# Fourier part folded along channels, woven into the second batch's output products; identity loaded first; row statistics on ScalarE

## The chip, the core and the metric

The kernel runs on one core of a Trainium2 chip. A core has a matrix engine (TensorE, PE in the rows), VectorE (DVE), ScalarE (ACT), GpSimd (POOL) and SyncE (SP), which here issues all transfers. Each engine takes its instructions in order; they wait for each other through semaphores. TensorE writes to PSUM, eight banks of 512 f32 columns; GpSimd cannot read PSUM. The metric is the device time of one execution in microseconds, lower is better.

## What is computed

Three stages follow each other, for two batches of 768 positions and 512 channels. The first is an attention with hashed buckets (8 heads of 64). The second gates a convolution. The third, which the change touches, is this:

```
gate = sigmoid(causal depthwise convolution of x, 5 taps)
x    = (gate * (x @ w_val)) @ w_out            # "y" in the kernel
X    = real(fft along channels (fft along the sequence (x)))
u    = x + X
un   = (u - mean(u)) / sqrt(var(u) + 1e-6)     # over the 512 channels
out  = u + relu(un @ w_ch1) @ w_ch2            # 512 -> 2048 -> 512
```

The real part of the two transforms is a sum of cosine and sine products: first along the sequence, then along the channels, with tables of cosines and sines as matrices.

## The kernel before

**Products.** Each f32 matrix product is made of three matmuls in the rounded type fp32r: both operands are cut into a high part (a copy that rounds) and a low part (the rest), and high x high, low x high and high x low are summed in PSUM (`three`, L1206, issued by `product`, L1087, so that nearly all matmuls have line L1090). So each operand costs a copy, mostly on ScalarE (`hi_...`), and a subtraction, on VectorE or GpSimd (`lo_...`).

**Stages.** The attention runs in 96 units, with `g` counting from -23 (`FIRST`); in it TensorE makes scores in a ring of three pairs of PSUM banks (L1193 to L1204), which VectorE's `maximum` (L827) frees. VectorE's queue before the first maximum holds a wait for the identity and its conversion to bf16 (L901 to L903). SyncE issues that load at `g == -12` (L471), after the first two sets of operands have been stacked and right after the loads of `qk` 2 and 3. After the attention come `values` (L1209), eight column groups for each batch, and `outputs` (L1223), six row tiles of 12 matmuls for each batch. VectorE multiplies with the gate (`gate_values`, L936) and cuts the low part (`lo_gv`, L927). `outputs` needs the first four `g_lo` of its batch for tiles 0 to 2, and all eight for tiles 3 to 5 (L1226).

**Transforms.** `fold_tile` makes sums and differences of the two sequence halves, for batch 0 on VectorE (L950), for batch 1 on GpSimd (L569); `hi_fold` (L722) and `lo_fold` (L578) cut them. `along_sequence` (L1237) runs eight tiles of 9 matmuls with 386 or 384 columns for a batch, `hi_seq` (L731) and `lo_seq` (L959) cut the spectrum, and `along_channels` (L1253) runs six row tiles of 24 matmuls with 258 or 256 columns. For its first tile it issues three quarters of the work before it waits for the last part of the spectrum (L1260). `add_mixed` (L965) adds the result to y in four pieces and takes `bn_stats`; `variances` (L982) and `inverse_deviations` (L992) give the scale, `normed` (L1007) gives `un`, which TensorE transposes (`turn_un`, L1268) and `hi_un` (L746) and `lo_un` (L1015) cut.

**Order and weights.** The order on each queue is written out: TensorE L1282 to L1304, VectorE L1022 to L1054, ScalarE L754 to L783, GpSimd L611 to L626. The Fourier tables come in 16 chunks that GpSimd cuts (`split_tables`, L599), from the end of the attention on. Then come the 16 chunks of w1: GpSimd cuts chunks 0 to 9 alone (`split_w1`, L602), and of the last six ScalarE makes the high part (`hi_w1`, L775) and GpSimd the low one (`lo_w1`, L605). SyncE loads a chunk when the one two before has been cut (L493), into two buffers. The feed-forward (`feed_block`, L1330) runs four blocks of 16 steps: `hidden`, 12 matmuls of 384 columns, and `project`, 9 of 512. Its first block needs all three `unt_lo`.

## Time and profile before

| | |
|---|---|
| time, median of 3 runs | 714.03 us (714.02 to 714.39) |
| time of the profiled execution | 714.04 us |
| its span, first to last instruction | 712.2 us |
| TensorE busy | 684.7 us, 96% |
| VectorE / ScalarE / GpSimd busy | 388.9 / 243.8 / 203.0 us |
| mean granted TensorE clock | 0.987 of full |

The span is read from the first to the last instruction, so 1.8 us of the execution lie around it. A matmul's recorded duration is longer than its place in the stream, as matmuls overlap: the distance between two starts, the pitch, is what a matmul costs. "Idle before" names what ended an engine's idle time. Several instructions of a kind in a row are merged, with their count behind an x.

### The profile page before, as it was taken

The numbers are of one execution on the slowest core, as the hardware profiler recorded it, in microseconds if no ns is written. First come the engines' busy times: TensorE is split into PE (matmuls) and PEld (weight loads), VectorE is DVE, ScalarE is ACT, GpSimd is POOL, SyncE is SP. The second block draws the span as 40 slices with busy tenths as digits, with TensorE's granted clock in tenths as the row PEclk, the third lists the DMA queues.
The fourth block names the chain that finished last, engine by engine and source line by source line (L and its number), as shares of the span: only waits on it lengthen the run. The fifth ranks groups of instructions, "written<-read, shape, count | busy, mean of one in ns | idle before, by whom it ended". The sixth has DMA issues, their size and how long they took to land.

```text
span 712.2 us, 10036 instructions
## 1 busy us (share of the span) xinstructions
PE 684.7 (96%) x3600; PEld 614.7 (86%) x3600; DVE 388.9 (55%) x621; ACT 243.8 (34%) x376; POOL 203.0 (29%) x193
## 2 busy tenths in 40 slices
PE   3699999999999999999999999999999999999998
PEld 2588888888888888798989999999999999999997
DVE  3566768888888888958745796321222122212112
ACT  2065545555555455654345241111112111211110
POOL 0001323232323233538848965880000000000000
PEclk9699999999999999999999999999999999999999
DMA  5945565555655441212202132330100010001001
GB/s 152 249 134 142 131 173 139 166 149 156 154 157 154 119 123 53 75 39 57 55 30 60 31 90 89 89 90 0 45 0 0 0 44 0 0 0 44 1 1 44
DMA packets 43846, 57.64 MB, mean 81 GB/s; under 512 B 21520, under 2 KB 25872, under 8 KB 43808
## 3 DMA queue, kind: packets, MB, share of 16 engines
q1 hardware_dynamic: 43808, 57.14, 29.0%
q8 instruction: 23, 0.38, 0.2%
q14 instruction: 15, 0.12, 0.1%
HBM read 31.81 MB, written 3.24 MB: 49 GB/s over the span
## 4 chain that ended last, share of the span: by engine, by line
PE 92%; DVE 3%; ACT 1%; DMA 1%; SPq 1%; issue 1%; DVEq 0%
PE psum L1090 74%; PE psum L1175 5%; PE psum L1176 4%; PE psum L1182 1%; PE psum L1183 1%; PE psum L1184 1%; PE psum L1187 1%; PE psum L1188 1%; PE psum L1185 1%; PE psum L1157 1%; DVE max_col L830 1%; PE psum L1278 1%; DMA ident<-in_ident_in 1%; DMA qk_raw<-in_qk 1%; ACT probs L669 1%
## 5 line engine op out<-in xcount | busy, mean ns | idle before, releaser
L1061 DVE SCALAR_TENSOR_TENSOR h_lo<-psum,h_hi 128x384 fp32r<-128x384 f32 x64 | 35.7, 558 | 184.2 <-ACT h_hi L791 184.2
L830 DVE TENSOR_REDUCE max_col<-psum 128x1 f32<-128x768 f32 x96 | 91.2, 953 | 40.8 <-PE psum L1090 40.6
L791 ACT ACTIVATE h_hi<-psum 128x384 fp32r<-128x384 f32 x64 | 31.5, 492 | 215.4 <-PE psum L1090 215.4
L669 ACT ACTIVATE probs<-psum 128x768 f32<-128x768 f32 x96 | 77.6, 809 | 39.8 <-PE psum L1090 39.8
L1090 PE MATMUL psum<-unt_hi,w_hi 128*128 (+1 forms) x256 | 86.9, 339 | 0.0
L1090 PE MATMUL psum<-unt_lo,w_hi 128*128 (+1 forms) x256 | 86.3, 337 | 0.0
L1090 PE MATMUL psum<-unt_hi,w_lo 128*128 (+1 forms) x256 | 85.9, 336 | 0.0
L1090 PE MATMUL psum<-a1k,a1q 128*128 128x384 f32 x192 | 67.9, 354 | 11.8 <-DVE max_col L830 6.7
L1090 PE MATMUL psum<-a1q,a1k 128*128 128x384 f32 x192 | 76.0, 396 | 0.8 <-ACT a2q L657 0.8
L1090 PE MATMUL psum<-w_lo,h_hi 128*128 128x512 f32 x192 | 75.9, 395 | 0.0
L1090 PE MATMUL psum<-w_hi,h_lo 128*128 128x512 f32 x192 | 75.8, 395 | 0.0
L1090 PE MATMUL psum<-w_hi,h_hi 128*128 128x512 f32 x192 | 74.6, 389 | 0.0
L1090 PE MATMUL psum<-a2k,a2q 96*128 96x384 f32 x192 | 67.2, 350 | 0.0
L546 POOL TENSOR_TENSOR vl<-v,vh 128x384 fp32r<-128x384 f32 x16 | 20.5, 1284 | 156.7 <-issue 81.6
L1090 PE MATMUL psum<-a2q,a2k 99*128 99x384 f32 x192 | 65.0, 339 | 0.0
L666 ACT ACTIVATE p_hi<-psum 128x768 fp32r<-128x768 f32 x48 | 39.0, 813 | 65.2 <-PE psum L1090 63.5
L836 DVE TENSOR_TENSOR p_lo<-probs,p_hi 128x768 fp32r<-128x768 f32 x48 | 54.0, 1125 | 3.2 <-ACT probs L669 3.2
L557 POOL TENSOR_TENSOR xT<-sums,rec_b 64x768 f32<-64x768 f32 x16 | 30.0, 1872 | 79.0 <-DMA rec_b<-rec_dram 74.4
L1090 PEld LDWEIGHTS psum<-unt_hi,w_hi 128*128 128x128 f32 x256 | 48.1, 188 | 2.2
L1090 PEld LDWEIGHTS psum<-unt_hi,w_lo 128*128 128x128 f32 x256 | 48.1, 188 | 2.2
L1090 PEld LDWEIGHTS psum<-a1k,a1q 128*128 128x128 f32 x192 | 38.2, 199 | 13.3 <-DVE max_col L830 7.3
L1090 PEld LDWEIGHTS psum<-unt_lo,w_hi 128*128 128x128 f32 x256 | 48.0, 188 | 0.0
(129 smaller groups left out, 1449.6 us busy)
## 6 DMA issues: line engine op xcount, KB each, us to landing
stg_w<-in_w SPq DMA_DIRECT2D x32, 256.0 KB, 2.6
qk_raw<-in_qk SPq DMA_DIRECT2D x16, 384.0 KB, 5.1
a1k<-qk_hi SPq DMA_DIRECT2D x32, 192.0 KB, 3.3
flag_b<-flag_dram SPq DMA_DIRECT2D x16, 384.0 KB, 4.2
a1q<-qk_hi SPq DMA_DIRECT2D x16, 192.0 KB, 2.8
a2q<-qk_hi SPq DMA_DIRECT2D x16, 192.0 KB, 3.5
a1q<-qk_lo SPq DMA_DIRECT2D x16, 192.0 KB, 3.7
a2k<-qk_lo SPq DMA_DIRECT2D x16, 192.0 KB, 3.7
```

The lines of the kernel that those rows point to most:

```text
L546: pool.tensor_tensor(vl[par][:, :].rearrange("p (t d) -> p t d", d=P), split_tiles(v1[par][:, :]), bits(vh[par][:, :]).rearrange("p (t d) ...
L557: pool.tensor_tensor(xT[rows, slot * S:(slot + 1) * S], sums[par][rows, :], rec_b[rows, :], ALU.mult).then_inc(x_ready, 1)
L666: act.activation(halves(p_hi[k % PHBUF][:, 0:S]), ring("st", i), ACT.Exp, scale=SCALE).then_inc(p_hi_ready, 1)
L669: act.activation(halves(probs[i % PBUF][:, 0:S]), ring("st", i), ACT.Exp, scale=SCALE).then_inc(probs_ready, 1)
L791: act.activation(h_hi[:, (j % 2) * HALF:(j % 2 + 1) * HALF], psum[:, j % 2, 0:HALF], ACT.Relu).then_inc(h_hi_ready, 1)
L830: dve.tensor_reduce(max_col[:, i % T:i % T + 1], ring("s", i), AX.XY, ALU.max).then_inc(max_done, 1)
L836: dve.tensor_tensor(p_lo[i % PBUF][:, 0:S], probs[i % PBUF][:, 0:S], bits(p_hi[k % PHBUF][:, 0:S]), ALU.subtract).then_inc(p_lo_ready, 1)
L1061: dve.scalar_tensor_tensor(h_lo[:, half], psum[:, j % 2, 0:HALF], 0.0, bits(h_hi[:, half]), ALU.max, ALU.subtract).then_inc(h_lo_ready, 1)
L1090: mm = pe.matmul(dst, lhs, rhs, start=first and n == 0, stop=last and n == len(pairs) - 1)
L1157: mm = pe.matmul(out_ps[0:MPARTS, t // HT, (t % HT) * P:(t % HT + 1) * P], neg_parts[:, MPARTS * t:MPARTS * (t + 1)], ident_b[:, :], start ...
L1175: pe.matmul(first, v1[par][:, w], probs[i % PBUF][:, 0:HALF], start=start, stop=stop)
L1176: pe.matmul(last, v1[par][:, w], probs[i % PBUF][:, HALF:PCOLS], start=start, stop=stop).then_inc(pv_done, 1)
```

## The change

The Fourier transform along the channels uses that a cosine is even and a sine is odd. After the sequence fold, each tile is folded once more along its 512 channels: channel c plus channel 512 - c (for the cosines) and minus it (for the sines), in a buffer `cf` with four places. So the sequence transform works on 2 x 256 folded channels, cosines and sines apart, with 194 or 192 columns instead of 386 or 384 and as many matmuls, and the channel transform has two channel tiles instead of four. Channel 0, which has no partner, is carried by itself: `fold_zero` on VectorE, 12 matmuls with two columns of weights for each batch, `hi_zero` and `lo_zero`, and one matmul with a row of ones at the end of each channel tile. All folds are on VectorE, those of batch 0 between the gate products of batch 1.

The order is new. The outputs come in the order 0, 3, 1, 4, 2, 5 (`Y_ORDER`), so that each pair of them gives the two tiles of a fold. After two outputs of batch 1 the whole sequence transform of batch 0 runs, and the other four outputs stand between its channel tiles, two and two. The identity is loaded before the first unit. The sums and the squares of a row come from two ScalarE activations with an accumulated output and a small one between them (`statistics`), instead of `bn_stats` and `bn_aggr` on VectorE. GpSimd cuts the first four chunks of w1 between the folds of batch 1. The buffers are laid out anew, and the tables have 210 columns a chunk instead of 274.

The diff, cut to its core:

```diff
+NE = HALF // 2 + 2
 NO = HALF // 2
 EV, OD = 2 * NE, 2 * NO
+CM = CT // 2
+CH = C // 2
...
+Y_ORDER = (0, 3, 1, 4, 2, 5)
+FOLDS = (0, 3, 1, 4, 2, 5)
+NCF = 4
+
+SEQ = ((0, 0), (1, 0), (0, 1), (1, 1))
+SEQ_BANK = ((0, 1, 2, 3), (6, 4, 5, 7))
+ZERO_BANK = (6, 2)
+OUT_BANK = (4, 5, 7)
...
+            sp.dma_start(ident[:, :], ident_in).then_inc(ident_loaded, 16)
...
+            for k in range(T):
+                lo_fold(0, k)
+            pool.wait_ge(val_done, 2 * CT * B)
+            lo_fold(1, 0)
+            lo_fold(1, 1)
+            split_w1((0, W1_EARLY // 4))
+            lo_fold(1, 2)
+            lo_fold(1, 3)
+            split_w1((W1_EARLY // 4, W1_EARLY // 2))
+            lo_fold(1, 4)
+            lo_fold(1, 5)
             pool.wait_ge(y_done, B * T)
-            split_w1((0, W1_EARLY // 2))
-            fold_tile(1, 0)
-            pool.wait_ge(seq_done, 2 * CT)
-            lo_fold(1)
             split_w1((W1_EARLY // 2, (W1_N - W1_LATE) // 2))
+            pool.wait_ge(seq_done, len(SEQ) * B)
             for chunk in range(W1_N - W1_LATE, W1_N):
                 lo_w1(chunk)
             pool.wait_ge(ch_done, B * T)
...
+            def hi_spectrum(b):
+
+                hi_seq(b, 0)
+                hi_seq(b, 1)
+                hi_zero(b)
+                if b > 0:
+                    statistics(b - 1, T - 2)
+                hi_seq(b, 2)
+                if b > 0:
+                    statistics(b - 1, T - 1)
+                hi_seq(b, 3)
+
+            def statistics(b, t):
+
+                n = T * b + t
+                u_t = y3[:, n, :]
+                act.wait_ge(u_step, 4 * (n + 1))
+                if n > 0:
+                    act.wait_ge(stats_ready, n)
+                act.activation(squares[:, :], u_t, ACT.Copy, accum_out=stats[:, 0, n:n + 1]).then_inc(stats_step, 1)
+                act.wait_ge(stats_step, 2 * n + 1)
+                act.activation(stats[:, 1, n:n + 1], stats[:, 0, n:n + 1], ACT.Copy, scale=-1.0 / C).then_inc(stats_step, 1)
+                act.wait_ge(stats_step, 2 * n + 2)
+                act.activation(squares[:, :], u_t, ACT.Square, bias=stats[:, 1, n:n + 1], accum_out=stats[:, 2, n:n + 1]).then_inc(stats_ready, 1)
...
+            for i in range(2 * CT):
+                hi_gv(1, i)
+                if i < T:
+                    hi_fold(0, i)
+            copy_y(1, 0)
+            copy_y(1, 1)
+            hi_spectrum(0)
+            for k in range(2, T, 2):
+                hi_fold(1, k - 2)
+                hi_fold(1, k - 1)
+                copy_y(1, k)
+                statistics(0, k - 2)
+                copy_y(1, k + 1)
+                statistics(0, k - 1)
+            hi_fold(1, T - 2)
+            hi_fold(1, T - 1)
+            hi_spectrum(1)
             deviations(0)
...
+                statistics(1, t)
...
+                n, f = T * b + k, FOLDS[k]
                 kt, odd = f % HT, f // HT
+                base = n % 2 * C
+                dve.wait_ge(y_ready, T * b + 2 * (kt + 1))
+                dve.tensor_tensor(fold[:, base:base + C], y3[:, T * b + kt, :], y3[:, T * b + kt + HT, :],
+                                  ALU.subtract if odd else ALU.add).then_inc(fold_ready, 1)
+                dve.wait_ge(fold_ready, n + 1)
+                if n >= NCF:
+                    dve.wait_ge(f_lo_ready, n - NCF + 1)
+                up, down = fold[:, base + 1:base + CH + 1], fold[:, base + C - 1:base + CH - 1:-1]
+                dst = cf[:, n % NCF * C:(n % NCF + 1) * C]
+                dve.tensor_tensor(dst[:, 0:CH], up, down, ALU.add).then_inc(cf_ready, 1)
+                dve.tensor_tensor(dst[:, CH:C], up, down, ALU.subtract).then_inc(cf_ready, 1)
...
-                dve.wait_ge(u_step, 4 * (n + 1))
-                dve.bn_stats(stats[:, n, :], u_t).then_inc(stats_ready, 1)
...
+            for i in range(2 * CT):
+                gate_value(1, i)
+                if i < T:
+                    fold_tile(0, i)
             lo_gv(4 * CT - 1)
-            for f in range(T):
-                fold_tile(0, f)
-            for n in range(2 * CT):
-                lo_seq(0, n)
-            for t in range(T):
-                add_mixed(0, t)
+            fold_zero(0)
+            fold_tile(1, 0)
+            lo_spectrum(0)
+            fold_tile(1, 1)
+            add_mixed(0, 0)
+            add_mixed(0, 1)
+            fold_tile(1, 2)
+            fold_tile(1, 3)
+            add_mixed(0, 2)
+            add_mixed(0, 3)
+            fold_tile(1, 4)
+            fold_tile(1, 5)
+            fold_zero(1)
+            add_mixed(0, 4)
+            add_mixed(0, 5)
+            lo_spectrum(1)
             variances(0)
-            for n in range(2 * CT):
-                lo_seq(1, n)
-                if n == 0:
-                    inverse_deviations(0)
+            inverse_deviations(0)
...
+            def along_sequence(b, k):
+
+                m, odd = SEQ[k]
+                n, base = (NO, WB_OD) if odd else (NE, WB_EV)
+                if k == 0:
+                    pe.wait_ge(gv_ready, 2 * CT * B)
+                    pe.wait_ge(y_ready, T * (b + 1))
+                pe.wait_ge(f_lo_ready, T * b + T - 1 + odd)
+                for a in range(2):
                     for kt in range(HT):
-                        f = slice((HT * odd + kt) * C + m * P, (HT * odd + kt) * C + (m + 1) * P)
-                        w = slice(base + kt * cols, base + (kt + 1) * cols)
-                        product(psum[:, n % 4, 0:cols], three(f_hi[:, f], f_lo[:, f], wb_hi[:, w], wb_lo[:, w]),
-                                done=seq_done if kt == HT - 1 else None, first=kt == 0, last=kt == HT - 1)
+                        at_ = (HT * odd + kt) * C + a * CH + m * P
+                        f, w = slice(at_, at_ + P), slice(base + (2 * kt + a) * n, base + (2 * kt + a + 1) * n)
+                        product(psum[:, SEQ_BANK[b][k], a * n:(a + 1) * n], three(f_hi[b][:, f], f_lo[:, f], wb_hi[:, w], wb_lo[:, w]),
+                                done=seq_done if a and kt == HT - 1 else None, first=kt == 0, last=kt == HT - 1)
+
+            def zero_along_sequence(b):
+
+                pe.wait_ge(y0_ready, b + 1)
+                if b > 0:
+                    pe.wait_ge(u_step, 4 * T * b)
+                for odd, n, base in ((0, NE, WB_EV), (1, NO, WB_OD)):
+                    for kt in range(HT):
+                        f, w = slice(2 * (HT * odd + kt), 2 * (HT * odd + kt + 1)), slice(base + 2 * kt * n, base + (2 * kt + 1) * n)
+                        product(psum[0:2, ZERO_BANK[b], odd * NE:odd * NE + n], [(y0_parts[:, f], wb_hi[:, w]), (y0_parts[:, f], wb_lo[:, w])],
+                                done=y0_done if odd and kt == HT - 1 else None, first=kt == 0, last=kt == HT - 1)
...
+            def spectra(b):
+
+                along_sequence(b, 0)
+                along_sequence(b, 1)
+                zero_along_sequence(b)
+                along_sequence(b, 2)
+                along_sequence(b, 3)
...
+                for m in range(CM):
+                    if t == 0:
+                        pe.wait_ge(seq_lo_ready, 2 * (len(SEQ) * b + 3 + m))
                     for a, base, cols in ((0, WB_COS, NC_), (1, WB_SIN, NS_)):
                         f = slice((2 * m + a) * S + t * P, (2 * m + a) * S + (t + 1) * P)
                         w = slice(base + m * cols, base + (m + 1) * cols)
-                        product(psum[:, 2 * (t % 3) + a, 0:cols], three(pq_t_hi[:, f], pq_t_lo[:, f], wb_hi[:, w], wb_lo[:, w]),
-                                done=ch_done if a and m == CT - 1 else None, first=m == 0, last=m == CT - 1)
+                        product(psum[:, bank + a, 0:cols], three(pq_t_hi[:, f], pq_t_lo[:, f], wb_hi[:, w], wb_lo[:, w]),
+                                first=m == 0, last=a == 1 and m == CM - 1)
+                if t == 0:
+                    pe.wait_ge(u0_lo_ready, 2 * (b + 1))
+                pe.matmul(psum[:, bank, 0:NC_], u0t[0:D, t * P:(t + 1) * P], ones_row[0:D, :], start=False, stop=True).then_inc(ch_done, 1)
...
+            output(1, 0)
+            output(1, 1)
             pe.wait_ge(wb_split, -(-WB_COS // WB_CH))
-            along_sequence(0)
+            spectra(0)
             pe.wait_ge(wb_split, NH)
-            pe.wait_ge(y_ready, B * T)
-            for t in range(T):
-                along_channels(0, t)
-            along_sequence(1)
+            pe.wait_ge(zeros_ready, 2)
+            along_channels(0, 0)
+            along_channels(0, 1)
+            output(1, 2)
+            output(1, 3)
+            along_channels(0, 2)
+            along_channels(0, 3)
+            output(1, 4)
+            output(1, 5)
+            along_channels(0, 4)
+            along_channels(0, 5)
+            spectra(1)
```

## Rows read from the trace of the kernel before

**Rows 1.** The page: busy time of the engines; the chain that ended last.
```profile
PE 684.7 (96%) x3600; PEld 614.7 (86%) x3600; DVE 388.9 (55%) x621; ACT 243.8 (34%) x376; POOL 203.0 (29%) x193
PE 92%; DVE 3%; ACT 1%; DMA 1%; SPq 1%; issue 1%; DVEq 0%
```
**Rows 2.** Windows by stage: length, busy us (records) per engine, granted clock, DMA share, GB/s.
```profile
358.00:374.30 16.30, 16.30 (x73) 13.45 (x72) 7.38 (x9) 6.73 (x12) 7.62 (x6) 1.00 0.10 32
374.30:387.00 12.70, 12.70 (x73) 12.70 (x72) 6.58 (x13) 6.97 (x15) 10.58 (x9) 1.00 0.24 67
387.00:404.50 17.50, 17.50 (x146) 17.38 (x146) 12.60 (x29) 5.78 (x9) 16.55 (x14) 1.00 0.04 13
404.50:418.60 14.10, 13.06 (x75) 12.74 (x74) 11.89 (x31) 6.25 (x15) 11.42 (x10) 1.00 0.32 94
418.60:437.20 18.60, 18.60 (x158) 18.49 (x157) 16.09 (x34) 6.08 (x11) 7.77 (x6) 1.00 0.33 100
```
**Rows 3.** Timeline of TensorE: start, us, engine, line, count, idle before and its end.
```profile
413.64 0.44 PE L1090 MATMUL psum<-wb_hi,f_hi 128*128 128x384 f32 x1 [1.04 <-DVE pq_t_lo L963]
...
443.45 0.33 PE L1090 MATMUL psum<-unt_hi,w_hi 128*128 x1
```
**Rows 4.** Weight loads of 128 and of 4 columns; plain f32 matmuls, merged, on the timeline.
```profile
L1090 PEld LDWEIGHTS psum<-x_lo,wa_hi 128*128 128x128 f32 x61 | 11.4, 188 | 0.0
L1157 PEld LDWEIGHTS psum<-ident_b,neg_parts x96: 80/84/85, 35.4 to 291.7; 128*4 128x4 bf16 x96
42.71 0.81 PE L1175 MATMUL psum<-probs,v 128*128 128x384 f32 x2
43.36 0.81 PE L1176 MATMUL psum<-probs,v 128*128 128x386 f32 x2
```
**Rows 5.** Timelines of SyncE, ScalarE and VectorE in the start.
```profile
21.48 0.43 SPq L471 DMA_DIRECT2D ident<-in_ident_in  x1
24.77 0.83 ACT L639 CAST qk_hi<-qk_raw 128x768 fp32r<-128x768 f32 x1 [11.18 <-DMA qk_raw<-in_qk]
26.13 0.23 DVE L903 CAST ident_b<-ident 128x128 bf16<-128x128 f32 x1 [13.41 <-DMA ident<-in_ident_in]
28.00 0.95 DVE L814 TENSOR_TENSOR qk_lo<-qk_raw,qk_hi 128x768 fp32r<-128x768 f32 x1
35.10 1.01 DVE L824 TENSOR_SCALAR hash_bits<-psum,pencol 128x768 f32<-128x768 f32 x1
```
**Rows 6.** Timeline of TensorE in the start; 13 matmuls start from 27.27 to 31.32.
```profile
16.41 0.69 PE L1090 MATMUL psum<-a1k,a1q 128*128 128x384 f32 x1 [4.75 <-DMA a2k<-hash_bits]
27.27 0.69 PE L1090 MATMUL psum<-a1k,a1q 128*128 128x384 f32 x1 [6.66 <-DVE max_col L830]
31.64 0.40 PE L1090 MATMUL psum<-a2k,a2q 96*128 96x384 f32 x1
```
**Rows 7.** First gate product and last table piece, timelines; VectorE's fold: duration ns min/median/max.
```profile
344.26 0.54 DVE L945 TENSOR_TENSOR gv<-gate,psum 128x384 f32<-128x384 f32 x1
354.84 0.88 POOL L597 TENSOR_TENSOR wb_lo<-stg_b,wb_hi 128x274 f32 x1 [0.17 <-POOL wb_hi L529]
L956 DVE TENSOR_TENSOR fold<-y x6: 679/684/1695, 359.8 to 369.0; 128x512 f32<-128x512 f32 x6
```
**Rows 8.** Groups by line and form, 310 to 450 us: busy us, mean ns, idle before.
```profile
L963 DVE TENSOR_TENSOR pq_t_lo<-psum,pq_t_hi 128x384 fp32r<-128x384 f32 x32 | 16.1, 553 | 13.6 <-ACT pq_t_hi L738 13.5
L738 ACT CAST pq_t_hi<-psum 128x384 fp32r<-128x384 f32 x32 | 14.3, 520 | 9.9 <-PE psum L1090 9.8
L585 POOL TENSOR_TENSOR f_lo<-fold,f_hi 128x512 fp32r<-128x512 f32 x12 | 15.3, 1291 | 9.3 <-ACT f_hi L729 9.3
L729 ACT CAST f_hi<-fold 128x512 fp32r<-128x512 f32 x12 | 7.3, 623 | 11.5 <-POOL fold L575 8.2 <-DVE fold L956 3.2
```
**Rows 9.** GpSimd's first piece of w1 chunk 4; ScalarE's last copy of the transposed `un`.
```profile
401.74 1.05 POOL L529 TENSOR_TENSOR w_hi<-stg_w,ones 128x512 f32 x1
432.18 0.58 ACT L751 CAST unt_hi<-psum 128x512 fp32r<-128x512 f32 x1
```

More of the change, by code:

```diff
@@ new lines, in copy_y, with hi_fold, hi_seq @@
+            def copy_y(b, k):
+                act.wait_ge(y_done, T * b + k + 1)
+                bank = OUT_BANK[k % 3] if b else 4 + k % 4
+                act.copy(y3[:, T * b + Y_ORDER[k], :], psum[:, bank, :]).then_inc(y_ready, 1)
+            def hi_fold(b, k):
+                n, f = T * b + k, FOLDS[k]
+                act.wait_ge(cf_ready, 2 * (n + 1))
+                act.copy(f_hi[b][:, f * C:(f + 1) * C], cf[:, (n % NCF) * C:(n % NCF + 1) * C]).then_inc(f_hi_ready, 1)
+            def hi_seq(b, k):
+                act.wait_ge(seq_done, len(SEQ) * b + k + 1)
+                if b == 0 and k == 0:
+                    act.wait_ge(val_done, 2 * CT * B)
+                if b > 0 and k == 0:
+                    act.wait_ge(ch_done, T * b)
+                for dst, src in spectrum(pq_t_hi, b, k):
+                    act.copy(dst, src).then_inc(seq_hi_ready, 1)
@@ L782, in _ @@
                     hi_w1(W1_N - W1_LATE + W1_LATE // HT * t + m)
+                statistics(1, t)
                 hi_un(0, t)
+            for t in range(HT, T):
+                statistics(1, t)
             def feed_block(r, first=False, last=False):
@@ L965, in add_mixed, with lo_spectrum @@
+            def lo_spectrum(b):
+                lo_seq(b, 0)
+                lo_seq(b, 1)
+                lo_zero(b)
+                lo_seq(b, 2)
+                lo_seq(b, 3)
             def add_mixed(b, t):
@@ L1023, in _ @@
             dve.wait_ge(x_ready, NH - 1)
-            gate_values(0, 0)
-            gate_values(0, 1)
+            for i in range(2 * CT):
+                gate_value(0, i)
             lo_gv(2 * CT - 1)
@@ L1221, in values @@
                                 done=val_done if c == CT - 1 else None, first=c == 0, last=c == CT - 1)
-            def outputs(b):
-                for t in range(T):
-                    pe.wait_ge(g_lo_ready, 2 * CT * b + CT * (t // HT + 1))
-                    if t >= 4:
-                        pe.wait_ge(y_ready, T * b + t - 3)
-                    elif b > 0:
-                        pe.wait_ge(y_ready, T * b)
-                    for c in range(CT):
-                        g = slice(c * S + t * P, c * S + (t + 1) * P)
-                        w = slice(CT * C + c * C, CT * C + (c + 1) * C)
-                        product(psum[:, 4 + t % 4, :], three(g_hi[:, g], g_lo[:, g], wa_hi[:, w], wa_lo[:, w]),
-                                done=y_done if c == CT - 1 else None, first=c == 0, last=c == CT - 1)
```

282 lines of the change are left out of this document (146 added, 136 removed).

## The prediction

> **What bounds the kernel now.** I read the page first: TensorE is busy in 96% of the span and the chain that ended last is 92% TensorE [rows 1]. So the kernel is a TensorE queue, and a change matters by the matmuls that it takes from that queue and the waits that it puts in. Next the table of stages [rows 2]. From 358.0 to 437.2 us TensorE runs, in this order, the outputs of batch 1 (72 matmuls of 512 columns, 16.3 us), the sequence transform of batch 0 (72 of 386 or 384 columns, 12.7), its channel transform (144 of 258 or 256, 17.5), and the same pair for batch 1 (14.1 and 18.6, the last with 12 transposes of `un`). One wait breaks it, 1.4 us around 413.6 [rows 3]; the feed-forward starts at 437.2 and its third `hidden` at 443.45 [rows 3]. VectorE and ScalarE are idle for a good part of every stage except where VectorE adds the spectrum. The third place is the start: TensorE idles 6.7 us before 27.27 [rows 6], while VectorE waits for the identity, whose load is issued only at 21.48 [rows 5].
>
> **The change part by part.** *Identity first.* SyncE issues it behind `pencol`, at about 2.6 us, where it otherwise waits until 4.7 for `qk_hi`; its 64 KB cost nothing there. VectorE then takes maxima 0 and 1 while scores 0 to 2 run, before 20.4. The next thing due on VectorE is `lo_qk(2)`, which needs `qk_hi`, ready at 24.77 + 0.83 = 25.6 because its load leaves SyncE just ahead of the identity's old place. Today it starts at 28.00 [rows 5]. VectorE is without a gap from there to the hash bits at 35.10, so this moves by 28.0 - 25.7 = 2.3 us. TensorE will again have idled some 5 us before scores 5 and start slow, which can take a part back: 1.2 to 2.3 gained. I take 2.3, since the VectorE row is the last one in the chain.
>
> *Matmuls removed.* The channel transform falls from 288 to 144 matmuls at 17.5/144 = 0.120 us (the stage's 146 records are 144 and two neighbours at its edges) [rows 2]: -17.3. The sequence transform keeps 144 matmuls, which shrink from 386/384 to 194/192 columns. No row has an operand of this rounded kind under 256 columns. From above, 258/256 columns take 0.120; from below, the slope between 512 columns (16.3/72 = 0.226) and 384 (0.176) is 0.4 ns a column, which gives 0.094 at 193. I take 0.120, because the weight load has a price of its own that narrow matmuls don't hide: 188 ns for 128 columns against 84 ns for 4, so 104 ns of it are columns [rows 4], and a stream of loads can't well go below it. Then 144 x (0.176 - 0.120) = -8.0; with 0.094 it is -11.8.
>
> The Trainium skill (TensorE: Matmul & The Clock Gate, LDWEIGHTS) puts a load at its columns divided by 1.2 GHz, 107 ns here; the two rows agree with it to 3 ns. As a floor of 107 it would make the sequence part 1.9 us shorter than my 0.120.
>
> *Matmuls added.* 24 with two columns of weights for channel 0, at 0.094 (no weight load to speak of; up to 0.120): +2.3. Twelve with a row of ones, 258 columns at 0.120: +1.4. Together TensorE loses 17.3 + 8.0 - 2.3 - 1.4 = 21.6 us of work.
>
> *What replaces it.* The folds move in front of the work that they feed. I followed each queue in order from 341 us, each instruction starting at the later of its engine and its last wait; pitches are the durations of [rows 8] less some 0.1 for overlap.
>
> (a) Between the outputs `output(1,0)` and `output(1,1)`. The second is now t = 3, so it needs all eight `g_lo` of batch 1. VectorE makes them in eight rounds from 344.26 [rows 7], and six rounds now also fold: alone 0.47 (gate value) + 0.47 (`g_lo`) + 0.60 (fold) + 2 x 0.34 (sum, difference) + 0.2 for two waits on its own results = 2.4. All but the first read two SBUF operands, and GpSimd is busy beside them: tables, whose last piece begins at 354.84 [rows 7] (16 chunks of 210 columns instead of 274 and two memsets, so about the same end), then `f_lo` at 1.29 each. Such an operation caught behind GpSimd takes 1.7 us, not 0.68 (the fold's median and longest) [rows 7]. About one in three is caught: 3.25 a round, 6 x 3.25 + 2.7 for the two plain rounds and the last `g_lo` = 366.5. `output(1,0)` ends at 360.6, so TensorE waits 5.9 us, where it waits for nothing now. Bounds: 0 with no contention, 9 with each one caught.
>
> (b) The clock. After 4.75 and 6.66 us of idleness TensorE came back with 13 matmuls from 27.27 to 31.64, 0.336 us each against 0.173 later [rows 6], the level of 1.2 GHz instead of 2.4: about 2.0 lost. Wait (a) is longer than the shorter of these: +2.0 (0 if it shortens below; the rows show none between 1.4 and 4.7 us that could say from where on).
>
> (c) `along_channels(0,0)`. Its second channel tile needs the last spectrum tile: 0.2 + 0.92 (ScalarE, two pieces) + 1.02 (VectorE, two) after TensorE is done [rows 8]. Today 18 matmuls lie in front of that wait and hide it; now six do: +1.4, and for batch 1, where ScalarE has statistics in between, +2.1.
>
> (d) `along_sequence(1,0)` needs folds that need `output(1,5)`: copy 0.6, fold and sums 2.6, ScalarE 0.62, GpSimd 1.29, some signals: 5.9 us after it, of which two channel tiles (2 x 1.56) hide 3.1: +2.8. Taking the outputs apart is what makes it this small.
>
> (e) `un` waits for the variances, which stand behind all of `lo_spectrum(1)` and a table load: +1.1 at the first transpose. The statistics as such: 12 `bn_stats` and 12 `bn_aggr` leave VectorE, where nothing waited for them but this chain; on ScalarE a tile costs two passes of 0.6 and a small one, 1.65 with signals. No row has an accumulating pass: at least the plain copy's 0.62, at most perhaps 0.2 more.
>
> (f) The second weights w1. GpSimd splits chunks 4 to 9 from 401.74 [rows 9]. Now it must first finish `lo_fold(1,5)`, at 407.4 by (a) to (d). From there to the last `hi_un` today's chain takes 432.18 - 401.74 = 30.4 us [rows 9], in part because ScalarE is late for its first chunk. I count six chunks at 2.47 (two pieces and their signals), 14.8, and three rounds of two chunks with `hi_w1` on ScalarE at 4.6, 13.8; `statistics` and `hi_un` stand behind each round's chunks and fit beside the loads. So the last `hi_un` starts at 436.0, and the feed-forward at 437.3. TensorE waits 2.8 before the third transpose and 5.4 before the feed-forward, and after the latter is slow again: +2.0.
>
> *Sum.* Work -21.6; waits 5.9 + 1.4 + 2.8 + 2.1 + 1.1 + 2.8 + 5.4 = 21.5, less the 1.4 of today: +20.1; clock 2 x 2.0 = +4.0; start -2.3. In all +0.2. Against the profiled execution's 714.04 (712.2 of span and 1.8 around it; the median is 714.03) this is 714.2 us. So 21.6 us of TensorE work turn into waits of about the same length.
>
> **The rivals.**
> 1. *The gate loop keeps up.* If VectorE and GpSimd hinder each other less than I say, the wait (a) shrinks to between 0 and 3.5, the clock doesn't fall there, and all that follows, chain (f) too, moves by as much: 714.2 - 2.0 - 4 = about 708, at the best 706. For it: VectorE alone needs 2.4 a round, and would be through at 362. Against: it needs GpSimd out of the way, and the tables and `f_lo` fill most of these 22 us.
> 2. *Narrow matmuls cost by their columns*, 0.094: -3.7 of work, of which chain (f) gives back half: 712.3. For it the slope, against it the weight loads.
> 3. *The slower one: VectorE and GpSimd take turns throughout.* The place is the gate loop again. If each two-input operation waits for a whole one of GpSimd, rounds cost 3.8 to 4.3 and `output(1,1)` starts at 369.5 to 372.5. It decides from about 368, that is from 3.5 a round; each us of it arrives at the end through (d) and (f). 714.2 + 3 to 8: 717 to 722. For it: the longest fold, 1.7, is exactly a fold behind a whole `f_lo`. The Trainium skill (SBUF — State Buffer, two separate sides) says that the port pair is an exclusive lock for the full instruction and that the loser fully blocks; the fold's row agrees, while the tables' chunks in the trace cost less than that rule would.
> 4. *Narrow matmuls run as plain f32 ones do.* The probabilities' f32 matmuls are two records of 0.325 us for 384 columns [rows 4], four times the rounded kind by column. 193 columns would then take 0.33: 144 x 0.21 = +30, part of which hides waits: about 739. For it only that no narrow rounded matmul stands in the trace.
>
> That the change doesn't do what it says: the statistics leave VectorE, but no wait goes with them. This is within the forecast.
>
> **How the numbers follow.** Forecast 714.2, chance 0.34, its own range 711.5 to 716.5. Rival 1 0.25, rival 2 0.12, rival 3 0.22, rival 4 0.07. The range 707 to 720 leaves out rival 4 (0.07), the lower end of 1 (0.04) and the upper of 3 (0.06). A measurement here can tell 0.2% from no change, so the bounds are 712.6 and 715.5. Faster: 1, half of 2, 0.07 of the forecast = 0.38. Same: 0.20 of the forecast and 0.06 of 2 = 0.26. Slower: 3, 4 and 0.07 of the forecast = 0.36.
>
> **What would show it.** TensorE's first gap: its start after `ident_b` near 27 us moves by 2.3. The pitch of the 192-column matmuls: 0.120, 0.094 or 0.33. A gap of 5.9 us before the 13th matmul of batch 1's outputs, ended by `g_lo`, with 1.2 GHz behind it. A gap of 5.4 before the feed-forward, ended by `unt_lo`, in front of it `w_hi` waits on ScalarE. The first `hidden` near 437.3 - 2.3 = 435.0. The forecast is wrong if `output(1,1)` comes before 364 or after 368, if chain (f) is shorter than 4.5 a round, or if the accumulating passes cost clearly more than 0.8 us.

## The result, and the profile after

The changed kernel takes 719.72 us (median of 4; 718.90 to 720.75) against 714.21 for the kernel before in the same comparison: ratio 1.0077, 95% interval 1.0061 to 1.0093. It is slower by 5.5 us. The forecast was 714.2, within 707 to 720; so the range held it, by 0.3 us (one of the four runs lies outside, at 720.75), and the size was missed by 5.5. It lies outside the forecast's own range of 711.5 to 716.5 and inside the 717 to 722 of rival 3, which had a chance of 0.22. The profiled execution has a span of 717.6 us, where 712.2 stood before.

The page of the changed kernel, busy times and the chain that ended last; it answers [rows 1]:

```profile
PE 672.5 (94%) x3492; PEld 597.0 (83%) x3492; DVE 393.3 (55%) x623; ACT 257.4 (36%) x424; POOL 192.9 (27%) x189
PE 84%; DVE 6%; DMA 3%; ACT 2%; issue 2%; POOL 2%; SPq 1%; POOLq 0%; DVEq 0%
```

TensorE is busy for 12.2 us less in a span that is 5.4 us longer, so it idles 17.6 us more. Its share of the chain fell from 92% to 84%, and what it lost went to VectorE, transfers and GpSimd. Where the idle time lies is in the windows of the changed kernel (length, then busy us and records of TensorE, weight loads, VectorE, ScalarE, GpSimd; granted clock; DMA share, GB/s). They answer [rows 2]:

```profile
358.00:366.00 8.00, 2.22 (x11) 1.49 (x9) 7.80 (x15) 3.06 (x6) 2.77 (x3) 0.95 0.01 2
366.00:372.00 6.00, 6.00 (x16) 4.84 (x17) 0.42 (x4) 0.48 (x1) 0.00 (x0) 0.50 0.27 87
...
414.00:420.00 6.00, 3.99 (x31) 3.52 (x29) 2.89 (x8) 5.19 (x13) 4.76 (x5) 0.98 0.31 89
420.00:426.00 6.00, 5.89 (x32) 4.99 (x32) 5.89 (x8) 0.62 (x1) 4.59 (x5) 0.74 0.29 90
...
438.00:441.00 3.00, 0.23 (x1) 0.23 (x2) 1.35 (x3) 2.87 (x9) 0.79 (x1) 0.87 0.32 107
```

From 358 to 366 TensorE does 2.2 us of work while VectorE does 7.8; the six microseconds behind that go at half the clock. The second cluster runs from 402 to 441. The same gaps one by one, from the timeline of TensorE (the bracket is the idle time before the matmul and what ended it):

```profile
357.16 0.50 PE L1212 MATMUL psum<-wa_hi,g_hi 128*128 128x512 f32 x1 [1.38 <-DVE g_lo L1016]
365.99 0.79 PE L1212 MATMUL psum<-wa_hi,g_hi 128*128 128x512 f32 x1 [5.78 <-DVE g_lo L1016]
406.58 0.33 PE L1212 MATMUL psum<-wb_hi,f_hi 128*128 128x194 f32 x1 [1.77 <-POOL f_lo L612]
431.06 0.63 PE L1425 MATMUL psum<-ident,un 128*128 128x128 f32 x4 [2.06 <-DVE unt_lo L1133]
440.77 0.68 PE L1212 MATMUL psum<-unt_hi,w_hi 128*128 x1 [5.44 <-DVE y L1091]
```

The last row is the feed-forward's first hidden. The semaphore of `y` that the row names had been met since 437.1; what came last was the third `unt_lo`, 439.65 to 440.34.

One round of the gate loop on VectorE, the last of the six with a fold, and then the GpSimd row that lies beside it:

```profile
359.51 0.55 DVE L1028 TENSOR_TENSOR gv<-gate,psum 128x384 f32<-128x384 f32 x1
359.98 0.55 DVE L1016 TENSOR_TENSOR g_lo<-gv,g_hi 128x384 fp32r<-128x384 f32 x1
360.44 1.75 DVE L1039 TENSOR_TENSOR fold<-y 128x512 f32<-128x512 f32 x1
362.23 0.42 DVE L1046 TENSOR_TENSOR cf<-fold 128x256 f32<-128x256 f32 x1
362.58 0.42 DVE L1047 TENSOR_TENSOR cf<-fold 128x256 f32<-128x256 f32 x1
362.91 0.55 DVE L1028 TENSOR_TENSOR gv<-gate,psum 128x384 f32<-128x384 f32 x1
```
```profile
360.39 1.26 POOL L612 TENSOR_TENSOR f_lo<-cf,f_hi 128x512 fp32r<-128x512 f32 x1 [2.14 <-ACT f_hi L764]
```

The fold starts 0.05 us behind `f_lo`, waits out its 1.26 and then takes its usual half microsecond: 1.75 instead of 0.68. In the last three rounds it repeats by itself: `f_lo` becomes due when ScalarE has rounded the last sum, and that is when VectorE reaches the next fold.

The six rounds, from 341.25 to 362.91, take 2.56, 3.62, 3.63, 5.03, 3.42 and 3.40 us, 3.61 on average. The first three lie beside the tables, whose pieces last 0.5 to 0.9 us; there the folds take 0.68, 1.12 and 1.12. The fourth is the longest, because GpSimd, done with the tables, has three `f_lo` to catch up with (VectorE, then GpSimd):

```profile
352.63 1.77 DVE L1039 TENSOR_TENSOR fold<-y 128x512 f32<-128x512 f32 x1
354.44 1.40 DVE L1046 TENSOR_TENSOR cf<-fold 128x256 f32<-128x256 f32 x1
```
```profile
350.82 4.74 POOL L612 TENSOR_TENSOR f_lo<-cf,f_hi 128x512 fp32r<-128x512 f32 x3
```

### The profile page after: what moved, and what is told of

The parts are those of the page before. It is cut to its first block, busy times and chain, and to the rows that moved or that the text cites. A ratio compares the mean times of both kernels' runs of the same rounds, so it can differ in the third digit from the quotient of the medians.

```text
span 717.6 us, 9860 instructions
## 1 busy us (share of the span) xinstructions
PE 672.5 (94%) x3492; PEld 597.0 (83%) x3492; DVE 393.3 (55%) x623; ACT 257.4 (36%) x424; POOL 192.9 (27%) x189
## 4 chain that ended last, share of the span: by engine, by line
PE 84%; DVE 6%; DMA 3%; ACT 2%; issue 2%; POOL 2%; SPq 1%; POOLq 0%; DVEq 0%
PE psum L1212 67%; PE psum L1297 5%; PE psum L1298 4%; DMA stg_w<-in_w 2%; DVE fold L1039 1%; PE psum L1304 1%; PE psum L1305 1%; PE psum L1306 1%; PE psum L1310 1%; PE psum L1309 1%; DMA qk_raw<-in_qk 1%; PE psum L1307 1%; PE psum L1279 1%; DVE cf L1047 1%; DVE g_lo L1016 1%
```

## The experiments

Times are given as ratios to the kernel before, which ran beside each; 0.0014 is 1 us. All but `e1_ident` and its repeat start from the changed kernel. Positions in a trace are those of one execution, which can lie 1 to 2 us from the median of its kernel (`e5_warm` 719.52 against 717.94, `e8_gated` 715.64 against 717.51); the gains are read from the ratios.

**The identity alone** (the kernel before, with the load moved).

```diff
+            sp.dma_start(ident[:, :], ident_in).then_inc(ident_loaded, 16)   # behind pencol
-                    sp.dma_start(ident[:, :], ident_in).then_inc(ident_loaded, 16)   # behind load_qk(3)
```

> The kernel before with one edit: the identity is loaded behind pencol. Theory: VectorE is free for lo_qk(2) at 25.7 instead of 28.0 and TensorE follows, so everything behind moves by 2.3 to 2.4 us and nothing is given back: 711.8 us. Rival: the longer idleness of TensorE ahead of scores 5 or a later transfer takes a part back: 712.8 or more.

712.31 us, ratio 0.9977 (0.9968 to 0.9987). The same kernel again in a later comparison, as `e12_ident_again`:

> The kernel of e1_ident once more, beside the last variant: 711.8 to 712.3 us, the time that a version with the Fourier part folded has to beat.

712.68 us, 0.9977 (0.9968 to 0.9986). The gain is 1.6 us, and its interval of 0.9 to 2.3 touches what I had taken. The first `qk_lo` moved a little further than forecast, to 25.15 and in the repeat to 25.59 instead of 25.7 (28.00 in [rows 5]):

```profile
25.15 0.96 DVE L814 TENSOR_TENSOR qk_lo<-qk_raw,qk_hi 128x768 fp32r<-128x768 f32 x1 [4.78 <-ACT qk_hi L639]
27.03 0.69 PE L1090 MATMUL psum<-a1k,a1q 128*128 128x384 f32 x1 [4.72 <-DVE max_col L830]
```

In the two profiles the end of the attention moved by 2.2 and 1.5 us (`sums`, 308.50 before, 306.28 here, 307.04 in the repeat). TensorE still idles 4.7 us and comes back slow. So the step stood, and 1.6 of the 2.3 us that I had taken arrived.

**f_lo of batch 0 on VectorE.**

```diff
             for i in range(2 * CT):
                 gate_value(1, i)
+                if 1 <= i <= T:
+                    lo_fold(0, i - 1)
                 if i < T:
                     fold_tile(0, i)
```

> The changed kernel, with f_lo of batch 0 made by VectorE in the gate loop (each one a round after its fold) instead of by GpSimd. Theory: the loop's rounds of 3.6 us are made by waits behind GpSimd's instructions; a fold takes 1.75 instead of 0.68 because f_lo runs beside it. VectorE's own work grows by 0.6 a round, but the folds of the last three rounds shrink by 1.1: rounds of 3.0 once the tables are done, output(1,1) starts at about 364.6 instead of 365.99, and the kernel takes about 718.3 us. Rival: the rounds are VectorE's own work and its waits on ScalarE; then they grow by 0.6 to 4.2, output(1,1) starts at 369.5, and the kernel takes 723 us.

719.31 us, 1.0079 (1.0062 to 1.0096): no difference from the changed kernel that these intervals show, where the theory wanted 1.4 us. In the trace the loop does what the theory says. Once the tables are done, VectorE does 0.6 us more per round and the rounds are shorter:

```profile
358.37 0.55 DVE L1026 TENSOR_TENSOR gv<-gate,psum 128x384 f32<-128x384 f32 x1
...
359.30 0.68 DVE L1054 TENSOR_TENSOR f_lo<-cf,f_hi 128x512 fp32r<-128x512 f32 x1
359.90 0.69 DVE L1037 TENSOR_TENSOR fold<-y 128x512 f32<-128x512 f32 x1
...
361.30 0.55 DVE L1026 TENSOR_TENSOR gv<-gate,psum 128x384 f32<-128x384 f32 x1
```

2.93 us against 3.40, with the fold at 0.69. The rival (rounds of 4.2) falls. In the second and third round, beside the tables, VectorE carries the added work and they grow to 4.32 and 4.04; the fourth falls from 5.03 to 2.93, as GpSimd has nothing to catch up with. From the first `gv` to `output(1,1)` it is 23.1 us instead of 24.7, and `output(1,1)` starts at 364.64, as the theory has it. The first hidden starts 1.3 us earlier too (439.43). Behind it the two executions differ: the clock granted in the next 8 us is 0.65 here and 0.82 in the changed kernel, 2.8 and 1.4 us lost. So in these two traces most of the gain went there; whether that is so in every execution, no run shows.

**TensorE kept busy in wait (a).** Before `output(1,1)`, twice:

```diff
+                for c in range(CT):
+                    g = slice(c * S, c * S + P)
+                    w = slice(CT * C + c * C, CT * C + (c + 1) * C)
+                    product(psum[:, OUT_BANK[1], :], three(g_hi[:, g], g_lo[:, g], wa_hi[:, w], wa_lo[:, w]),
+                            first=c == 0, last=c == CT - 1)
```

> The changed kernel with 24 matmuls more, on TensorE, in the 5.8 us in which it waits for g_lo before output(1,1): two times the products of output(1,0), written to the bank that output(1,1) then starts afresh. They last 5.4 us at full clock, so they fit. Theory: the granted clock stays at 1.00, the 13 matmuls behind the wait take 0.23 instead of 0.43 us each, along_sequence(0,0) starts 2.5 us earlier, and most of it arrives at the end: 717.4 us. Rival: the time behind the wait is set by VectorE and ScalarE and not by these matmuls: 719.2 to 719.9 us.

717.94 us, 1.0055 (1.0038 to 1.0072), 1.6 us below the changed kernel by the ratios, 1.8 by the medians, though the two intervals overlap; `e10_all` below adds the same matmuls to another kernel, and there they don't. The windows of TensorE (busy, granted clock); in the changed kernel the same two have 0.22 us at 0.93 and 6.00 at 0.50:

```profile
360.00:366.00 6.00, 6.00 (x28) 1.00 0.00 0
366.00:372.00 6.00, 5.56 (x34) 1.00 0.28 87
```

From `output(1,0)` to the second channel tile it is 23.1 us instead of 25.7.

**The statistics back on VectorE.**

```diff
+                dve.bn_stats(stats[:, n, :], u_t).then_inc(stats_ready, 1)      # behind the sums of add_mixed
-                statistics(1, t)                                                # ahead of hi_un(0, t) on ScalarE, and the others
```

> The changed kernel with the row statistics back on VectorE (bn_stats behind the sums, bn_aggr in the variances), as in the kernel before. Theory: on ScalarE they cost little on the path: hi_w1 of chunks 12 and 14 starts about 0.8 us earlier, the first project 0.3; VectorE gives back up to 0.6 at batch 1's folds. 718.2 us, between 717 and 720. Rival: the statistics on ScalarE are what the change loses by; then the feed-forward starts 4 us or more earlier: 715.5 or less.

718.06 us, 1.0063 (1.0046 to 1.0080), 1.0 us better by the ratios, with intervals that overlap. That is what the theory said (718.2); the rival, 715.5 or less, falls. TensorE's waits in this kernel:

```profile
424.66 1.11 PE L1410 MATMUL psum<-ident,un 128*128 128x128 f32 x4 [2.29 <-DVE un L1109]
431.63 0.63 PE L1410 MATMUL psum<-ident,un 128*128 128x128 f32 x4 [0.78 <-DVE unt_lo L1118]
438.66 0.69 PE L1197 MATMUL psum<-unt_hi,w_hi 128*128 x1 [2.74 <-DVE y L1070]
```

The waits of 2.06 and 5.44 shrink to 0.78 and 2.74, and one of 2.29 appears at the first transpose: the first `un` starts at 424.06 instead of 422.37, after 0.5 us of aggregation and three instructions on six columns that take 0.95 to 1.19 us beside GpSimd's, where the changed kernel has two of that kind. The statistics on ScalarE are a part of the loss, about 1 us at most as these runs show it, and not its main part.

**f_lo of both batches on VectorE**, so that GpSimd can split w1 chunk 4 at once.

```diff
-            lo_fold(1, 0)                         # ... to lo_fold(1, 5) leave GpSimd's queue
-            lo_fold(1, 1)
-            split_w1((0, W1_EARLY // 4))
+            pool.wait_ge(seq_done, len(SEQ))
+            split_w1((0, W1_EARLY // 2))
```

> The changed kernel with f_lo of both batches made by VectorE. GpSimd then splits w1 chunks 0 to 3 as soon as batch 0's sequence transform is done, and chunk 4 as soon as the last output product is read, at about 401 instead of 408.8. Theory: the feed-forward waits for chain (f), which begins behind lo_fold(1,5) on GpSimd; with it gone the waits of 2.1 before the third transpose and of 5.4 before the feed-forward go, and the slow clock behind them: 708 to 710 us. Rival: the feed-forward would wait as long for ScalarE (statistics, hi_un) or for the transfers of w1: 715 us or more.

722.86 us, 1.0119 (1.0102 to 1.0136). It is 3 us slower than the changed kernel, which neither side had: the theory misses, and the rival names a wait that is there (5.04 us before the feed-forward) but not the one that costs the 3 us. GpSimd's row first, then VectorE's:

```profile
411.10 1.51 POOL L624 TENSOR_TENSOR w_lo<-stg_w,w_hi 128x512 f32 x1 [0.17 <-POOL w_hi L565]
```
```profile
408.53 1.50 DVE L1039 TENSOR_TENSOR cf<-fold 128x256 f32<-128x256 f32 x1
409.96 1.52 DVE L1048 TENSOR_TENSOR f_lo<-cf,f_hi 128x512 fp32r<-128x512 f32 x1
411.40 1.23 DVE L1057 TENSOR_TENSOR y_raw<-y 128x3 f32<-128x3 f32 x1
412.55 0.15 DVE L1058 TENSOR_TENSOR y_raw<-y 128x3 f32<-128x3 f32 x1
```

An instruction on three columns takes 1.23 us where its twin takes 0.15: it ends at 412.63, as `w_lo` does at 412.61. Chunk 4 did start early, at 401.53, but `along_sequence(1,0)` then waits 6.78 us for VectorE (1.77 in the changed kernel), and the feed-forward starts at 444.84 instead of 440.77.

**The same, with w1 chunk 4 behind the last f_lo.**

```diff
             pool.wait_ge(y_done, B * T)
+            pool.wait_ge(f_lo_ready, B * T)
```

> The kernel of e3_floboth with one wait more: GpSimd begins w1 chunk 4 only when VectorE has made all twelve f_lo. Theory: e3 lost because chunks 4 to 9 ran beside the last folds of batch 1, where each two-input instruction of VectorE waits out one of GpSimd's; kept apart, the four instructions of a fold take 0.68 and 0.42 again instead of 1.2 to 1.8, the wait before along_sequence(1,0) falls from 6.8 to 1 us or less, chunk 4 starts at 406 instead of 408.8, and the kernel takes 716.5 us (715.5 to 718). Rival: VectorE simply has too much work at this place; then the wait stays above 3 us and the time above 719.

717.51 us, 1.0045 (1.0028 to 1.0062). One added wait takes 5.3 us off e3_floboth, within the theory's 715.5 to 718. Chunk 4 starts at 404.64. The fold beside an idle GpSimd (its two sums take 0.42 each), and TensorE's wait:

```profile
400.99 0.69 DVE L1032 TENSOR_TENSOR fold<-y 128x512 f32<-128x512 f32 x1
```
```profile
403.22 0.33 PE L1223 MATMUL psum<-wb_hi,f_hi 128*128 128x194 f32 x1 [0.62 <-DVE f_lo L1049]
```

The rival, too much work on VectorE, falls. The waits behind this place stay, 2.18 before the third transpose and 4.15 before the feed-forward.

**The same as e3_floboth, with the statistics on VectorE too.**

> The changed kernel with f_lo of both batches on VectorE and the statistics there too. Theory: with chain (f) started early, ScalarE's statistics between hi_w1 and hi_un are the next thing late; taking them away gains 1 to 2 us more than f_lo alone: 707 to 708 us. Rival: VectorE, with 12 f_lo and 12 bn_stats more, becomes late with its folds and sums: 710 us or more, slower than with the statistics left on ScalarE.

717.72 us, 1.0049 (1.0032 to 1.0065). It keeps the wait of 6.78 us of e3_floboth, which neither expectation had in it, and is 5 us faster than that kernel all the same. With w1 early, the feed-forward of e3_floboth waits 5.04 us for `hi_un` behind the statistics. They cost more there than their own 1.8 us: the statistics of batch 1's first tile need its sums, and while ScalarE waits for these, the next `hi_un` and the late chunks of w1 stand behind it.

```profile
432.37 0.63 ACT L797 ACTIVATE squares<-y 128x512 f32<-128x512 f32 x1 [4.84 <-DVE y L1099]
```

The next two `hi_w1` start at 434.56 there, and the last two at 439.64 and 440.89, behind their transfers; in e7_comb they start at 429.39, 430.72, 434.09 and 435.68, and the wait before the feed-forward is small:

```profile
439.90 0.43 PE L1207 MATMUL psum<-unt_hi,w_hi 128*128 x1 [1.52 <-DVE y L1072]
```

So what the statistics cost depends on whether chain (f) hides them: 1 us in the changed kernel, 5 where w1 is split early. The theory's 707 to 708 is missed by 10, for the wait of 6.78; that VectorE would be slower with the statistics than without them falls.

**Batch 1's outputs in the order 0, 1, 3, 4, 2, 5.**

```diff
+Y_ORDER_1 = (0, 1, 3, 4, 2, 5)
-            fold_tile(1, 0)                       # and fold_tile(1, 1): now behind add_mixed(0, 1)
             lo_spectrum(0)
```

> The changed kernel with batch 1's output products in the order t = 0, 1, 3, 4, 2, 5, so that the two ahead of the spectra need only the first four g_lo; the folds of tiles 0 and 1 move behind add_mixed(0,1). Theory: TensorE does output(1,1) at 359.9, then waits until the last gate value, about 364.6, and starts along_sequence(0,0) there instead of at 371.7: 6.8 us gained at this place. At the end little of it arrives, because GpSimd's queue of six lo_fold and four w1 chunks now starts at 388 instead of 380.7 and is the bound: 718 to 719 us. Rival: the wait before output(1,1) is what costs the time, and what is gained there arrives: 713 us.

720.08 us, 1.0083 (1.0066 to 1.0100), no better than the changed kernel. The wait before `output(1,1)` is gone, and one of 1.86 stands before the sequence transform; what was gained is lost again 40 us later, before the next one, for `f_lo` on GpSimd, as the theory said. The rival's 713 falls:

```profile
365.69 0.33 PE L1216 MATMUL psum<-wb_hi,f_hi 128*128 128x194 f32 x1 [1.86 <-issue]
408.10 0.50 PE L1216 MATMUL psum<-wb_hi,f_hi 128*128 128x194 f32 x1 [7.51 <-POOL f_lo L613]
```

**w1 chunks 8 to 11 early**, on e8_gated: their places hold the weights of the values, which are used up.

```diff
+W1_ORDER = (0, 1, 2, 3, 8, 9, 10, 11, 4, 5, 6, 7, 12, 13, 14, 15)
-W1_LATE = 2 * HT
+W1_LATE = 4
+            split_w1((2, 4), first=-4)            # 8 to 11, right behind 0 to 3
```

> The kernel of e8_gated with w1 chunks 8 to 11 split early as well: their destinations are free as soon as the values are computed, so GpSimd splits 0 to 3 and 8 to 11 from 381 to 401 us, 4 to 7 behind the last f_lo, and only 12 to 15 are left for the late rounds with ScalarE. Theory: the feed-forward waits for w1 and for nothing else as long; with 10 us less in chain (f) the waits of 2.1 and 5.4 us go, and the slow clock behind the second: 710.5 us (708.5 to 712.5). Rival: GpSimd, now busy in all of 381 to 401 us, holds VectorE up there, and the folds and sums come late: 715 us or more.

715.09 us, 1.0010 (1.0001 to 1.0020): 2.5 us gained over e8_gated; the theory's 710.5 is missed, and the time is the rival's. The wait before the feed-forward is gone, but GpSimd's eight chunks now lie beside the folds, and both sides of my expectation happened: the wait before `along_sequence(1,0)` grew from 0.62 to 2.08, and waits of 0.60 and 0.89 for VectorE's sums came into the channel tiles. The largest of them on TensorE:

```profile
406.64 0.34 PE L1230 MATMUL psum<-wb_hi,f_hi 128*128 128x194 f32 x1 [2.08 <-DVE f_lo L1056]
```

**With the filling matmuls** of e5_warm on top:

> The kernel of e9_early with the 24 filling matmuls of e5_warm. Theory: they gain what they gained there, 1.8 us, since nothing else hides it: 708.7 us. Rival: the time is set by VectorE and GpSimd from 381 us on, and the filling gains under 0.7 us.

712.56 us, 0.9981 (0.9971 to 0.9992): they gain 2.1 us here, with intervals apart. From `output(1,0)` to the second channel tile it is 22.3 us instead of 24.5. The granted clock from 420 to 427 is also higher, 0.87 against 0.53 in e9_early, so the gain need not all come from the filled wait. TensorE then waits for ScalarE twice:

```profile
433.30 0.44 PE L1230 MATMUL psum<-unt_hi,w_hi 128*128 x1 [1.41 <-DVE y L1101]
439.16 0.49 PE L1230 MATMUL psum<-w_hi,h_hi 128*128 128x512 f32 x1 [1.43 <-DVE h_lo L1201]
```

`h_hi` of the first hidden started at 437.96, behind the statistics of tiles 3 to 5.

**With ScalarE's order mended.**

```diff
-                statistics(1, t)
                 hi_un(0, t)
+                statistics(1, t)
...
-            for t in range(HT, T):
-                statistics(1, t)                  # now one behind h_hi(0), two behind h_hi(1)
```

> The kernel of e10_all with ScalarE's order around the feed-forward changed: the last four w1 chunks ahead of all statistics of batch 1, each hi_un ahead of the statistics of its tile, and the statistics of tiles 3 to 5 between the first h_hi. Theory: in e10_all the first hidden waits 1.4 us for the last unt_lo, which stood behind statistics(1,2), and the first project another 1.4 us for h_hi, which stood behind statistics(1,3) to (1,5); both waits go, and the kernel takes 710 us (709 to 711.5). Rival: the first project then waits as long for w2, whose first chunk is split at 435.5 us, or the variances come late for the second block: 712 us or more.

709.66 us, 0.9937 (0.9923 to 0.9951). It beats the kernel before by 4.5 us and the identity alone by 2.9. The two waits fell to one of 0.35, and the first project starts at 437.06 without one.

## Why the prediction was wrong in size

I set the changed kernel's times beside the forecast's, moved by the 2.3 us of the start. `output(1,1)`: 364.2 forecast, 365.99 measured, +1.8. GpSimd's chunk 4: 405.1 and 408.77, +3.7. Last `hi_un`: 433.7 and 439.06, +5.4. First hidden: 435.0 and 440.77, +5.8. What lies behind it gave 0.6 back, for +5.2 in the profiled execution (719.4 against 714.2). So each stage of this one path added something, and the forecast of a path was right: the gains did turn into the waits that it named. By its own signs it was just wrong at the first of these places, as `output(1,1)` came 0.3 us behind the 368 that it had as its latest.

The sum tells the same in its terms. TensorE lost about 18.3 us of matmul work (17.3 + 9.2 - 2.2 - 6.0, with the prices below) and not 21.6. The waits came to about 20 us (7.2, 1.3, 2.0, 1.8, 0, 2.1, 5.4 and one of 0.4 that I had not named) against 21.5. The clock cost about 5.6 us in three stretches against 4.0 in two. That the waits agree so well in total is in part luck: (a) was 1.3 too small, (d), (e) and the wait before the third transpose together 2.9 too large.

**Start, -2.3.** Right in the trace of the changed kernel (-2.3 at `sums`), 1.6 in the time of the identity alone.

**Matmuls, -21.6.** Too much. Sequence matmuls came at 0.112 (35 steps from 376.67 to 380.58) and not 0.120, another -1.2 over 144, and rival 2's 0.094 is out. It is the weights and not the columns that set it: the zero-channel matmuls stream the same 194 columns with two columns of weights and take 0.090. But the twelve ones matmuls were mis-sized: I had priced them at 0.120 each, like their neighbours. TensorE's matmuls, then its weight loads, of the changed kernel:

```profile
394.87 0.28 PE L1212 MATMUL psum<-wb_lo,pq_t_hi 128*128 128x256 f32 x1
395.07 0.38 PE L1413 MATMUL psum<-ones_row,u0t 64*128 64x258 f32 x1
395.39 0.50 PE L1212 MATMUL psum<-wa_hi,g_hi 128*128 128x512 f32 x1
```
```profile
394.75 0.19 PEld L1212 LDWEIGHTS psum<-wb_lo,pq_t_hi 128*128 128x128 f32 x1
395.07 0.18 PEld L1413 LDWEIGHTS psum<-ones_row,u0t 64*128 64x128 f32 x1
395.38 0.19 PEld L1212 LDWEIGHTS psum<-wa_hi,g_hi 128*128 128x128 f32 x1
```

The load for the matmul at 394.87 starts at 394.75, one matmul ahead. The one of 64 rows starts with its own matmul, and so does the one behind it. Thirteen matmuls from 393.45 take 1.94 us, where 13 x 0.120 is 1.56: each ones matmul costs 0.50. Twelve of them: 6.0 instead of 1.4. Four lie ahead of chain (f), which is +1.5 on the path. The Trainium skill (TensorE: Matmul & The Clock Gate, Step-by-step) says that a load is pulled ahead of running matmuls when the row groups don't conflict or when it goes to the background weight buffer, and that the time of a load doesn't depend on its rows. The time agrees: 0.18 us for 64 rows, 0.19 for 128. Which of the two conditions this load misses, the rows don't tell, since loads of 128 rows run ahead of matmuls that use all rows. Loads of 96 rows run ahead as well, here by 0.17 us, first the load and then its matmul:

```profile
69.39 0.19 PEld L1212 LDWEIGHTS psum<-a2k,a2q 96*128 96x128 f32 x1
```
```profile
69.56 0.34 PE L1212 MATMUL psum<-a2k,a2q 96*128 96x384 f32 x1
```

So among the forms of this kernel only the 64-row one isn't pulled ahead. That the number of rows is the reason is read from these rows and not tested: no run changed it, and the ones matmul is also the last of its group and adds to a bank of which the matmuls just before it wrote the neighbour.

**(a) +5.9.** Measured 1.38 + 5.78 = 7.2. Rounds took 3.61, not 3.25: six times 0.36, less 0.7 from an earlier first `gv` and plus 0.4 from a later last `g_lo`, is the +1.8. This is rival 3's side: it decides from 3.5 a round or 368 for `output(1,1)`, and on that axis it came at 368.3. Its mechanism holds throughout, its price of 3.8 to 4.3 a round doesn't, since a table piece is shorter than an `f_lo`. "About one in three is caught" was the wrong step: of the 23 instructions with two SBUF operands in these six rounds 14 took longer than alone, five of the six folds among them. I had treated being caught as chance; the fold and `f_lo` are tied to each other by their semaphores. e2_flo0 takes `f_lo` away and the fold is back at 0.69; e3_floboth and e8_gated show the same thing in both directions, with 5.3 us between them. The Trainium skill (SBUF — State Buffer, two separate sides) states this rule: an instruction of VectorE with two SBUF inputs and one of GpSimd that reads SBUF exclude each other for the whole instruction. I cited it and gave the case a chance of 0.22, on the ground that beside the tables' chunks the trace showed less. That was misread. In the kernel before (VectorE, then GpSimd) a `g_lo` that takes 0.55 alone starts with a piece of the tables and ends 0.41 us behind it:

```profile
352.37 1.04 DVE L933 TENSOR_TENSOR g_lo<-gv,g_hi 128x384 fp32r<-128x384 f32 x1
```
```profile
352.35 0.65 POOL L529 TENSOR_TENSOR wb_hi<-stg_b,ones 128x274 f32 x1 [0.64 <-DMA stg_b<-in_w_b]
```

It costs less only because the piece is shorter.

**(b) +2.0.** The clock stood at 0.50 to about 372; twelve matmuls from 365.99 to 371.28 took 5.3 us instead of 2.8, 2.5 lost. Filling the wait gained 1.6 us in e5_warm and 2.1 in e10_all, so the term is shown. Behind the wait before the feed-forward the clock was 0.82 over 8 us: 1.4 lost, not 2.0. A third slow stretch was not forecast: after 416 to 419, where TensorE was busy for 1.1 us of 3, with waits of only 0.59 and 1.42, the clock fell from 419.8 to 423.1, and 258/256-column matmuls took 0.215 instead of 0.120. That is some 1.6 us, though inside the wait for chain (f). In e5_warm the same two waits (0.58 and 1.43) stand at this place and the clock stays at 1.00, so they alone don't foretell it.

**(c) +1.4 and +2.1.** 1.3 and 2.0. **(d) +2.8.** 1.77. **(e) +1.1.** No wait was left at the first transpose, and TensorE, slow since 419.8, came there late itself. Today's wait, which the sum takes off as 1.4, is 1.04 in [rows 3]. The two accumulating passes of a tile take 0.63 + 0.19 and 0.73 + 0.19, with reading the accumulator as an instruction of its own, 1.8 us from the first to the last against my 1.65.

**(f) 28.6 us.** 30.3, and it began 3.7 us late. Six chunks took 16.3 and not 14.8, because the third and the fifth chunk waited 0.46 and 0.72 us for their transfers and the first `hi_w1` for its own; the three rounds took 14.0 and not 13.8. The prediction counts this chain as GpSimd's and ScalarE's work, and much of it is neither. w1 has two buffers, so a chunk is loaded only when the one two before is cut, and on the chain that ended last five transfers of 2.5 to 2.8 us make up 12.9 of the 30.3 us. Three of the longer pieces of that chain, with ScalarE's `w_hi` between the first two:

```profile
424.92 2.45 DMA stg_w<-in_w
428.09 1.28 POOL w_lo L635
429.54 2.59 DMA stg_w<-in_w
```

Whether a third buffer for w1 would shorten it, no run tried. e9_early shows that this chain was what the feed-forward waited for: with four chunks taken out of it the wait is gone.

Between `output(1,1)` and chunk 4 the path grew by another 1.9: +1.5 ones matmuls, +0.5 clock, -0.6 narrower pitch, and the rest, about 0.5, lies at the last two folds, where two sums took 1.39 and 1.48 beside `w_lo` and `f_lo`. That split is arithmetic from the trace, not an experiment.

## What to carry to other kernels

When VectorE and GpSimd both run instructions with two SBUF inputs, price each pair that the semaphores bring together as taking turns, the later one behind the whole of the earlier, not as an average; keep them apart by a wait if need be, which here was worth 5.3 us. Work taken off a full TensorE is gained only if the stage behind it was not already waiting: follow the queue that has the next thing due, here the loading and splitting of the weights, before counting matmuls. A matmul of another height than its neighbours can cost four of them; an idle TensorE of 5 us cost another 1.4 to 3 us afterwards in these traces, and idle time can be filled with matmuls that nobody reads.

## What was new about the hardware

- A weight load of 64 rows among loads of 128 wasn't overlapped with the matmul before it, nor was the one behind it: 0.50 us for one matmul against 0.12.
- Rounded matmuls of 192 columns with 128 columns of weights come at 0.112 us, with 2 columns of weights at 0.090.
- A 128x3 instruction of VectorE with two SBUF operands took 1.23 us behind one of GpSimd's, 0.15 without. Those with one operand in PSUM stayed at 0.41 to 0.55 beside a busy GpSimd.
- The clock fell without a long wait (none over 1.42 us), behind 3 us in which TensorE was busy for 1.1, in the changed kernel and not in e5_warm with the same two waits.
